# Attention scores per head on the two row halves of the array, and a small addition moved to ScalarE

## The reference, cut to what matters

```python
# q, k, v: 4 batches, 8 heads, 576 positions, 64 wide; window = 128
scores = scale * q @ k.T
rel = pos[:, None] - pos[None, :]
bias = slopes[head] * -abs(rel)                  # one slope a head
scores = where((rel >= 0) & (rel < window), scores + bias, -1e9)
attn = exp(scores - max(scores))
attn = attn / (sum(attn) + 1e-9)
x = attn @ v                                     # 2304 tokens x 512
x = (sigmoid(x @ w_gate) * (x @ w_val)) @ w_out  # d_ff 1536
out = ((x @ w1) * (x @ w2)) @ w3 @ w_out2        # d_ff 1024
```

## Time and profile before

| what | value |
|---|---|
| time, median of 3 runs | 971.4 us (971.06 to 971.5) |
| the profiled execution's own time | 972.31 us |
| its span | 970.5 us |
| TensorE busy | 899.5 us (93%) |
| VectorE busy | 689.1 us (71%) |
| ScalarE busy | 505.8 us (52%) |
| GpSimd busy | 722.3 us (74%) |
| first and last reciprocal L768 of attention start at | 16.7 and 231.7 us |

### The profile page before, as it was taken

How to read it: one execution, slowest core, us unless ns; L and a number is a source line. 1 busy time by engine, 2 the same in 40 slices (tenths; PEclk the granted TensorE clock), 3 DMA queues, 4 the chain that set the end, 5 groups by cost and what they waited for, 6 DMA issues and landing times.

```text
span 970.5 us, 15723 instructions
## 1 busy us (share of the span) xinstructions
PE 899.5 (93%) x5272; PEld 869.0 (90%) x5272; DVE 689.1 (71%) x1506; ACT 505.8 (52%) x1139; POOL 722.3 (74%) x535
## 2 busy tenths in 40 slices
PE   3999989868999997999999999799999999989998
PEld 3889877767899997899889999789988999988998
DVE  7988899885666668577756666857785666686666
ACT  4888878767544443544454444354444444435441
POOL 6778877876887775998679777489867977738940
PEclk9999999979999999999999999999999999998999
DMA  7333432410222210222142222012113211211301
GB/s 235 105 108 113 121 95 78 143 47 23 86 76 78 66 66 22 72 82 69 41 140 79 66 83 71 22 66 87 66 44 131 87 66 66 67 42 52 102 1 66
DMA packets 37409, 75.92 MB, mean 78 GB/s; under 512 B 3153, under 2 KB 16081, under 8 KB 37329
## 3 DMA queue, kind: packets, MB, share of 16 engines
q1 hardware_dynamic: 37328, 74.92, 23.9%
HBM read 68.09 MB, written 6.82 MB: 77 GB/s over the span
## 4 chain that ended last, share of the span: by engine, by line
PE 71%; DVE 14%; ACT 7%; issue 5%; POOL 2%; DMA 1%; SPq 0%; ACTq 0%; DVEq 0%; POOLq 0%
PE quad_ps L424 15%; PE quad_ps L426 14%; PE quad_ps L425 14%; PE o_ps L424 8%; PE o_ps L426 8%; PE o_ps L425 8%; DVE rowsum L766 3%; DVE xs_lo L811 2%; ACT exps L584 2%; DVE negs L755 1%; DVE xf L879 1%; POOL prob L1007 1%; ACT pt_hi L595 1%; DVE pt_lo L775 1%; ACT wq_hi L630 1%
## 5 line engine op out<-in xcount | busy, mean ns | idle before, releaser
L424 PE MATMUL quad_ps<-xs_hi,wq_hi 128*128 128x384 f32 x840 | 286.9, 342 | 25.4 <-ACT s L646 22.0
L426 PE MATMUL quad_ps<-xs_hi,wq_lo 128*128 128x384 f32 x840 | 284.6, 339 | 0.0
L425 PE MATMUL quad_ps<-xs_lo,wq_hi 128*128 128x384 f32 x840 | 284.5, 339 | 0.0
L424 PEld LDWEIGHTS quad_ps<-xs_hi,wq_hi 128*128 128x128 f32 x840 | 160.8, 191 | 31.7 <-issue 16.5
L1041 POOL TENSOR_TENSOR wq_lo<-wsum,wq_hi 128x1280 fp32r<-128x1280 f32 x60 | 177.3, 2955 | 9.4 <-ACT wq_hi L630 9.4
L424 PE MATMUL o_ps<-h_hi,wo_hi 128*128 128x384 f32 x480 | 161.2, 336 | 3.2 <-DVE xf L879 3.1
L425 PEld LDWEIGHTS quad_ps<-xs_lo,wq_hi 128*128 128x128 f32 x840 | 160.7, 191 | 0.0
L426 PEld LDWEIGHTS quad_ps<-xs_hi,wq_lo 128*128 128x128 f32 x840 | 160.5, 191 | 0.0
L426 PE MATMUL o_ps<-h_hi,wo_lo 128*128 128x384 f32 x480 | 160.4, 334 | 0.0
L425 PE MATMUL o_ps<-h_lo,wo_hi 128*128 128x384 f32 x480 | 160.4, 334 | 0.0
L1037 POOL TENSOR_TENSOR wq_lo<-raw_q,wq_hi 128x512 fp32r<-128x512 f32 x60 | 77.7, 1295 | 105.8 <-ACT wq_hi L624 105.8
(11 more groups left out here) (89 smaller groups left out, 1893.8 us busy)
## 6 DMA issues: line engine op xcount, KB each, us to landing
raw_q<-w SPq DMA_DIRECT2D x24, 512.0 KB, 3.5
raw_q<-w_gate SPq DMA_DIRECT2D x18, 512.0 KB, 3.5
raw_q<-w_val SPq DMA_DIRECT2D x18, 512.0 KB, 3.5
raw_o<-w_out SPq DMA_DIRECT2D x18, 512.0 KB, 3.5
raw_o<-w_times_wout SPq DMA_DIRECT2D x12, 512.0 KB, 3.6
k_raw<-kT SPq DMA_DIRECT2D x16, 288.0 KB, 2.9
q_raw<-qT SPq DMA_DIRECT2D x16, 288.0 KB, 3.0
v_raw<-v SPq DMA_DIRECT2D x16, 256.0 KB, 2.7
```

What stands on the lines that cost most here:

```text
L424: pe.matmul(out, lh, rh, start=start, stop=False, skip_group_check=onto)
L425: pe.matmul(out, lh, rl, start=False, stop=False, skip_group_check=onto)
L426: return pe.matmul(out, ll, rh, start=False, stop=stop, skip_group_check=onto)
```

## The change

Scores are computed per head. A step has 128 queries (64 in the last step of a pair) and 256 keys; `q_hi` and `q_lo` are plain copies of q, without zeros. Each head's product runs on its own 64 partitions, that is on one half of the array's rows, into its own PSUM bank `pA[h]`; matmuls of the two heads alternate. Both banks are used in every step, so `scores(n)` waits for `scored` of step n-1 instead of n-2. The bias tile is twice as many heads by 256 instead of 192 columns. `negs`, `exps`, `prob` are laid out by head; exponentials, scores and normalise go over 256 keys (128 in the first step, 192 in the last). q's high part is one cast of all partitions on ScalarE, its low part one subtraction on GpSimd; VectorE's part of it is gone. The addition of 1e-9 is done by ScalarE right behind the exponentials; VectorE keeps the reciprocal alone. The last step of a pair has four transposes instead of two.

```diff
-KW = WINDOW + QB
+KW = WINDOW + P
@@ loads: the wait for q's split, and the bias
-                for split in q_split:
-                    wait(sp, split, p)
+                wait(sp, q_split, p)
@@ TensorE scores
-                wait(pe, scored, n - 1)
-                first = max(0, i - 1) * P
-                last = min(S, first + 2 * P)
-                for j in blocks_of(i):
-                    q = slice((2 * i + j) * P, (2 * i + j + 1) * P)
-                    mm = product(pA[buf][:, j * 2 * P:j * 2 * P + last - first],
-                                 (q_hi[pb][:, q], q_lo[pb][:, q]),
-                                 (k_hi[pb][:, first:last], k_lo[pb][:, first:last]))
+                wait(pe, scored, n)
+                keys, q = keys_of(i), slice(i * P, (i + 1) * P)
+                first, last = (i - 1) * P + keys.start, (i - 1) * P + keys.stop
+
+                sides = ((q_hi, k_hi), (q_hi, k_lo), (q_lo, k_hi))
+                for k, (left, right) in enumerate(sides):
+                    for h in range(2):
+                        rows = slice(h * D, (h + 1) * D)
+                        mm = pe.matmul(pA[h][:, keys], left[pb][rows, q], right[pb][rows, first:last],
+                                       start=k == 0, stop=k == 2)
@@ ScalarE
-                if i in (1, 2):
+                if i == 1:
                     act.wait_ge(q_in, 16 * (pair + 1))
-                    h = i - 1
-                    nc.scalar.copy(diagonal(q_hi[pb], h), blocks(q_raw, h)).then_inc(q_hi_done, 1)
+                    wait(act, qk_done, STEPS * (pair - 1))
+                    nc.scalar.copy(q_hi[pb][:, 0:S], q_raw[:, :]).then_inc(q_hi_done, 1)
...
                 op.then_inc(exp_done, 1)
+                act.wait_ge(exp_done, n + 1)
+                wait(act, recip_done, n - 1)
+                nc.scalar.activation(rowsum2[0:rows, 3 * buf:3 * buf + 2], rowsum[0:rows, 3 * buf:3 * buf + 2],
+                                     ACT.Identity, bias=tiny[0:rows, 0:1]).then_inc(sum_done, 1)
@@ VectorE
-                if i == 2:
-                    dve.wait_ge(q_hi_done, 2 * pair + 2)
-                    nc.vector.tensor_tensor(out=diagonal(q_lo[pb], 1), in0=blocks(q_raw, 1),
-                                            in1=diagonal(q_hi[pb], 1), op=ALU.subtract).then_inc(q_split[1], 1)
...
-                dve.wait_ge(exp_done, n + 1)
-                nc.vector.tensor_scalar(rowsum2[:, cols], rowsum[:, cols], 1e-9, None, ALU.add).then_inc(sum_done, 1)
                 dve.wait_ge(sum_done, n + 1)
@@ GpSimd
-                    pool.wait_ge(q_hi_done, 2 * pair + 1)
-                    nc.gpsimd.tensor_tensor(out=diagonal(q_lo[pb], 0), in0=blocks(q_raw, 0),
-                                            in1=diagonal(q_hi[pb], 0), op=ALU.subtract).then_inc(q_split[0], 1)
+                    pool.wait_ge(q_hi_done, pair + 1)
+                    nc.gpsimd.tensor_tensor(out=q_lo[pb][:, 0:S], in0=q_raw[:, :], in1=q_hi[pb][:, 0:S],
+                                            op=ALU.subtract).then_inc(q_split, 1)
```

More of the change, by code:

```diff
@@ L122, in build @@
             v_lo = [sb(one, f"v_lo{b}", [P, VC * P], F32R) for b in range(2)]
-            bias = sb(one, "bias", [P, HP * KW], F32)
+            bias = sb(one, "bias", [P, H * KW], F32)
             eye = sb(one, "eye", [P, P], F32)
@@ L126, in build @@
             exps = [sb(one, f"exps{b}", [P, 2 * KW], F32) for b in range(2)]
-            prob = [sb(one, f"prob{b}", [P, 2 * (2 * P + QB)], F32) for b in range(2)]
+            prob = [sb(one, f"prob{b}", [P, 2 * KW], F32) for b in range(2)]
             pt_hi = [sb(one, f"pt_hi{b}", [P, 4 * P], F32R) for b in range(2)]
@@ L201, in where, with rows_of, keys_of, heads @@
             return n // STEPS, n % STEPS
-        def blocks_of(i):
-            return (0, 1) if 2 * i + 1 < NQ else (0,)
+        def rows_of(i):
+            return min(P, S - i * P)
         def chunks_of(i):
             return (1,) if i == 0 else (0, 1)
[L211 to L225, removed]
+        def keys_of(i):
+            return slice(P if i == 0 else 0, P + rows_of(i))
+        def heads(ap):
+            return ap[:, :].rearrange("p (h c) -> p h c", h=2)
+        def bias_of(pair):
+            return bias[:, pair % HP * 2 * KW:(pair % HP + 1) * 2 * KW]
         def raw_block(r):
@@ L581, in exponentials @@
                 wait(act, norm_done, n - 1)
[L582 to L586, removed]
+                rows = rows_of(i)
+                for h in range(2):
+                    op = nc.scalar.activation(heads(exps[buf])[0:rows, h, keys_of(i)],
+                                              heads(negs[buf])[0:rows, h, keys_of(i)], ACT.Exp, scale=-1.0,
+                                              bias=negmax[0:rows, 2 * buf + h:2 * buf + h + 1],
+                                              accum_out=rowsum[0:rows, 3 * buf + h:3 * buf + h + 1])
                 op.then_inc(exp_done, 1)
+                act.wait_ge(exp_done, n + 1)
+                wait(act, recip_done, n - 1)
+                nc.scalar.activation(rowsum2[0:rows, 3 * buf:3 * buf + 2], rowsum[0:rows, 3 * buf:3 * buf + 2],
+                                     ACT.Identity, bias=tiny[0:rows, 0:1]).then_inc(sum_done, 1)
             def turned_hi(n):
@@ L751, in score @@
                 buf = n % 2
-                for j in blocks_of(i):
-                    skip = seen(i, j)
-                    first = j * 2 * P + (0 if i == 0 else j * QB)
+                rows, keys = rows_of(i), keys_of(i)
+                for h in range(2):
                     op = nc.vector.tensor_tensor_reduce(
-                        negs[buf][:, j * KW + skip:(j + 1) * KW], pA[buf][:, first:first + KW - skip],
-                        bias[:, pair % HP * KW + skip:(pair % HP + 1) * KW], -SCALE, 3.0e38, ALU.add, ALU.min,
-                        negmax[:, 2 * buf + j:2 * buf + j + 1])
+                        heads(negs[buf])[0:rows, h, keys], pA[h][0:rows, keys],
+                        heads(bias_of(pair))[0:rows, h, keys], -SCALE, 3.0e38, ALU.add, ALU.min,
+                        negmax[0:rows, 2 * buf + h:2 * buf + h + 1])
                 op.then_inc(scored, 1)
```

75 lines of the change are left out of this document (33 added, 42 removed).

## The result

The changed kernel takes **991.0 us** (median of 4 runs, 990.52 to 991.84) against 971.3 us before: a ratio of **1.0204** (95% interval 1.0186 to 1.0221), 19.7 us slower. The forecast was 977 us, slower by 5.7. The direction is right, the size is not: the loss is more than three times the sum.

What follows compares the result with a forecast made beforehand. No engine alone bounded attention; L766's wait for GpSimd lay on the chain, and ScalarE would lead after the change. Pairs 1 to 8 +5.7, pairs 9 to 15 -1.8, start +1.8: +5.7 us, 977 us, range 962 to 992.

Steps and rivals of the forecast that it cites:

- the wait for the step before: TensorE's scores, attention: next scores at best 1.0 us later, reciprocal needs 1.5, so the wait is hidden in the loop.
- The small addition: New on ScalarE behind the exponentials: 0.40 us a step (bounds 0.25 and 0.50), 2.0 us a pair.
- the 102.4 of the sum: ScalarE's need over pairs 1 to 8: 84.78 + 8 x 2.2 = 102.4 us.
- the sum with a leading engine at 97% and 93%: Attention: ScalarE leads, busy 97% of pairs 1 to 8 and 93% of pairs 9 to 15.
- Exponentials and scores: Wider instructions in attention: exponentials on ScalarE 0.10 us more a full step, VectorE's scores 0.14 us more a step.
- The loop: Attention, from step to step: 2.03 + 0.44 = 2.47 us, below ScalarE's need per pair.
- halfway between the bounds: TensorE's score matmuls of a full step: 0.70 us, between 0.36 side by side and 1.02 with mode changes.
- The start: Larger bias load ahead of the first weight block: 1.8 us more, from 0 to 3.1.
- The sums: Attention stretches: pairs 1 to 8 take 105.5 us (+5.7), pairs 9 to 15 take 101.6 (-1.8).
- The switch of the array: Slower rival, TensorE: each change between half and full array costs 0.16 us; 984 us, chance 0.20.
- The prediction's port wait: Faster rival, VectorE: L766's waits for GpSimd, 36 us, nearly all on the chain, go; 963 us, chance 0.30.
- the effects cancel: Rival, attention loop: L766's 36 us come back as the small addition's 32 us; 971 us, chance 0.15.

Runs made afterwards that it cites:

- a_small1: The changed kernel with the addition of 1e-9 moved from ScalarE to VectorE, one instruction a column: 991.4 us, ratio 1.0197.
- b_small_act: The kernel before with only the small addition of 1e-9 moved to ScalarE behind the exponentials: 967.7 us, ratio 0.9951.

## Why the prediction was wrong in size

**The step that failed** is the wait for the step before. The prediction named it, named what is queued behind it (values, transposes, fold, ScalarE's copies), and then costed it at nothing: the next scores come 1.0 us after the last, the reciprocal needs 1.5, so the wait is hidden in the loop. That compared one chain with another for an undisturbed step. It left out two things. First, all that follows the scores on TensorE moved from one slot ahead to the same slot as VectorE's; so every wait that reached into TensorE's slot, and had been slack for that reason alone, became real. The cast of v is one (15.7 us; 9 us of time when taken away). Second, the lead is what carries TensorE over a late VectorE, and VectorE is late often: the wait for its scores came 42 times for 22, and behind a 3.23 us sum TensorE stood 2.73 us. The clock that fell there is a small part: with the single wait alone half of the loss came at full clock, and with the lead given back the clock was as low (0.88 from 138 to 235 us) while 13 us returned. The single wait costs 34 us alone, 17 us with the addition on ScalarE (967.7 to 984.6), and 13 us came back when the changed kernel got its lead.

**The other terms.** *The small addition*: 0.30 us long, started 0.62 us behind the second exponential (93.33 to 93.95), as said; it holds ScalarE's next instruction back by about 0.34 us instead of 0.40. *ScalarE* is busy for 98.33 us in pairs 1 to 8; the 102.4 of the sum held the gaps around the addition, which are not busy time. But its load did not set the pace: taking the addition off it changed nothing (a_small1), so the sum with a leading engine at 97% and 93% was built on the wrong bound: ScalarE was busy for 91% and 81%. *Exponentials and scores* over 256 keys: 503 and 417 ns, as worked out.

```profile
L578 ACT ACTIVATE exps<-negs,negmax 128x256 f32<-128x256 f32 x96 | 48.1, 503 | 6.8 <-DVE negmax L749 5.4 <-POOL prob L995 1.4
L585 ACT ACTIVATE rowsum<-rowsum,tiny 128x2 f32<-128x2 f32 x64 | 19.0, 297 | 2.1
L749 DVE CUSTOM_DVE_ANT_0 negs<-score_ps,bias 128x256 f32<-128x256 f32 x96 | 36.5, 417 | 0.0
```

*The loop* in the last steps turns in 2.42 us (242.71 to 245.13), forecast 2.47. *TensorE's scores*: 0.55 us, and 0.11 on the next product, and 0.08 ahead of them where no wait hides it, for 0.70; the halves side by side and the cost of the switch nearly cancel, as "halfway between the bounds" had it by luck. *The start*: +1.9 us for +1.8, by luck as well. The addition on ScalarE alone makes the start 2.1 us shorter (26.39 for 28.46), which the sum had at nothing, and the new layout with its bias then makes it 4.0 longer (26.42 to 30.38), not 1.8. *The sums*: pairs 1 to 8 took 107.90 us for 105.5, pairs 9 to 15 took 113.00 for 101.6. The second is the larger miss. I had taken VectorE's relief to lift the busiest engine from 84% to 93%; it fell to 81%. The single wait alone loses 17.9 us in that stretch.

**The rivals.** The switch of the array, at 984 us, is refuted as a cause: its price is seen, up to 0.4 us a step, but the halves run side by side and give it back, and all rows are no faster (992.8). The prediction's port wait, that of L766 for GpSimd, was real, 13.5 us in the kernel before; it could have made the change faster, and did as far as it goes (b_small_act, 967.7). That the effects cancel did not happen: the cancelling term was not ScalarE's load but the lost lead.

**Open** is how the 6.4 us between 984.6 and 991.0 divide between bias and layout: 4.0 lie at the start, where the larger bias load stands, and 2.4 in pairs 9 to 15; but the bias was split only in a form that loads less than before. And why VectorE's addition over two columns waits for GpSimd while one column does not was not tried beyond these two shapes.

## What to carry to other kernels

When a change takes a buffer from a pipelined loop, list every wait in every engine's program that points at the engine which loses its lead, not only the wait that the diff edits: slack that rests on running a slot ahead goes all at once. Compare chains for the worst step too (the one with the long instruction), not only for an undisturbed one. And when an instruction of a few elements shows a mean far above its shortest, look at what runs on the neighbour engine while it lasts, and try another shape of the same instruction before moving it to a third engine.

## What the runs showed of the hardware

A VectorE addition of a constant over 128x2 waits for a running GpSimd instruction (726 ns on average over 64, up to 2.34 us), the same over 128x1 does not (147 ns on average over 144, at most 156). The sums with two operands in SBUF wait too (L793 3.23 us, L800 2.21 us, where the one at 135.3 us in the changed kernel takes 0.94). Two matmuls on the two row halves into two banks run fully side by side, 0.28 us for both, and entering and leaving that mode costs about 0.4 us together when nothing waits. TensorE's clock fell to 1.2 GHz behind a standstill of 2.73 us and came back some 6 us after work had resumed (157.13 to 163.1 us).
